# Attention and two expert layers on one core: first steps rearranged, and value products issued ahead of the next step's transposes

## The reference

```python
# q, k, v: (2, 8, 768, 64)   n_global = 8, n_local = 96
scores = (q @ k.T) / 8 - slope[h] * dist          # dist from position, n_local for global keys
scores = where(is_global | is_local, scores, -1e9)
a = softmax(scores);  x = (a @ v) -> (1536, 512)  # rows: batch and position, columns: heads
P = sinkhorn(exp(x @ w_gate))                     # 8 rounds over 1536 x 8
y = sum_e P[:, e] * (relu(x @ w1[e]) @ w2[e])     # 8 experts, 512 -> 1024 -> 512
out = one expert per row of y, 192 rows each, chosen in order of the logits
```

## Time and profile before

| what | value |
|---|---|
| median of 3 runs | 1588.49 us (1587.71 to 1588.54) |
| profiled execution | 1589.48 us, its span 1587.7 us |
| granted TensorE clock, mean over the span | 0.926 |
| busy share: TensorE, its weight loads, VectorE, ScalarE, GpSimd | 91%, 75%, 41%, 22%, 12% |
| chain that ended last, by engine | TensorE 87%, VectorE 7%, issue 3%, ScalarE 2% |
| share of that chain in L1232 to L1234 (expert layers) | 26%, 25%, 26% |
| L572, exponentials | 41.8 us in 96 |
| L829, bias | 34.5 us in 96 |

### The profile page before, as it was taken

How to read it: one execution, slowest core, us unless ns; L and a number is a source line. 1 busy time by engine, 2 the same in 40 slices (tenths; PEclk the granted TensorE clock), 3 DMA queues, 4 the chain that set the end, 5 groups by cost and what they waited for, 6 DMA issues and landing times.

```text
span 1587.7 us, 19242 instructions
## 1 busy us (share of the span) xinstructions
PE 1437.2 (91%) x7340; PEld 1187.6 (75%) x7340; DVE 655.0 (41%) x1572; ACT 343.6 (22%) x522; POOL 187.6 (12%) x176
## 2 busy tenths in 40 slices
PE   7997999999999999999999999999999233389997
PEld 4876788888888888888888888888886222278886
DVE  4365543232332332323323233232333888746663
ACT  2475212011021121211112202112112000034442
POOL 2242211011010110101101011010010200021210
PEclk7599999999999999999999999999999555589999
DMA  5552111010110101101011010010110300036660
GB/s 122 146 139 75 54 53 53 0 53 0 53 53 0 53 0 53 53 0 53 1 52 53 0 53 26 27 53 0 53 53 0 132 0 0 0 130 219 211 215 20
DMA packets 80021, 91.74 MB, mean 58 GB/s; under 512 B 36976, under 2 KB 43120, under 8 KB 79984
## 3 DMA queue, kind: packets, MB, share of 16 engines
q1 hardware_dynamic: 75024, 84.26, 16.7%
q0 software_dynamic: 2048, 6.29, 1.3%
q10 hardware_dynamic: 2912, 0.72, 0.3%
HBM read 84.97 MB, written 6.29 MB: 57 GB/s over the span
## 4 chain that ended last, share of the span: by engine, by line
PE 87%; DVE 7%; issue 3%; ACT 2%; POOL 0%; ACTq 0%; DMA 0%; DVEq 0%; POOLq 0%
PE PS L1232 26%; PE PS L1234 26%; PE PS L1233 25%; PE PS L1198 3%; PE PS L1324 2%; DVE G L989 1%; PE PS L1169 1%; PE PS L1179 1%; ACT sc L572 1%; PE PS L1246 0%; DVE xlo L849 0%; DVE thr L987 0%; PE PS L1347 0%; DVE lo L1000 0%; PE PS L1112 0%
## 5 line engine op out<-in xcount | busy, mean ns | idle before, releaser
L1232 PE MATMUL PS<-xhi,w1hi 128*128 128x512 f32 (+1 forms) x1024 | 372.0, 363 | 4.6 <-DVE hlo L855 3.2
L1233 PE MATMUL PS<-xlo,w1hi 128*128 128x512 f32 (+1 forms) x1024 | 370.8, 362 | 0.0
L1234 PE MATMUL PS<-xhi,w1lo 128*128 128x512 f32 (+1 forms) x1024 | 370.7, 362 | 0.0
L1232 PE MATMUL PS<-w2hi,hhi 128*128 128x512 f32 (+1 forms) x896 | 349.5, 390 | 0.0
L1234 PE MATMUL PS<-w2hi,hlo 128*128 128x512 f32 (+1 forms) x896 | 349.3, 390 | 0.0
L1233 PE MATMUL PS<-w2lo,hhi 128*128 128x512 f32 (+1 forms) x896 | 349.0, 390 | 0.0
L611 ACT ACTIVATE hhi<-PS 128x512 fp32r<-128x512 f32 (+1 forms) x256 | 135.6, 531 | 903.3 <-PE PS L1234 903.3
L855 DVE SCALAR_TENSOR_TENSOR hlo<-PS,hhi 128x512 fp32r<-128x512 f32 (+1 forms) x256 | 155.3, 607 | 409.3 <-ACT hhi L611 409.0
L868 DVE SCALAR_TENSOR_TENSOR acc<-PS,prob_e,acc 128x512 f32<-128x512 f32 x192 | 144.1, 750 | 352.2 <-PE PS L1234 352.0
L1232 PEld LDWEIGHTS PS<-xhi,w1hi 128*128 128x128 f32 x1024 | 194.8, 190 | 38.2 <-DVE hlo L855 4.0
L1233 PEld LDWEIGHTS PS<-xlo,w1hi 128*128 128x128 f32 x1024 | 194.8, 190 | 30.7
(11 more groups left out here) (193 smaller groups left out, 901.8 us busy)
## 6 DMA issues: line engine op xcount, KB each, us to landing
raw<-in_w SPq DMA_DIRECT2D x64, 1024.0 KB, 5.4
x_rows<-acc SPq DMA_DIRECT2D x3, 1024.0 KB, 10.6
vs<-in_v SPq DMA_DIRECT2D x14, 192.0 KB, 3.0
vw<-in_v SPq DMA_DIRECT2D x14, 120.0 KB, 2.9
qs<-in_qT SPq DMA_DIRECT2D x4, 384.0 KB, 4.0
kp<-in_kT SPq DMA_DIRECT2D x4, 384.0 KB, 4.9
raw<-in_qT SPq DMA_DIRECT2D x4, 384.0 KB, 4.2
raw<-in_kT SPq DMA_DIRECT2D x4, 384.0 KB, 5.0
```

The source lines that it names most:

```text
L1232: T.matmul(o, whi, xh, start=first, stop=False)
L1233: T.matmul(o, whi, xl, start=False, stop=False)
L1234: return T.matmul(o, wlo, xh, start=False, stop=last)
```

## The change

Three things. In the start: v of head 0 is loaded by SP, behind q and k of head 0 and ahead of q and k of head 1, instead of by ScalarE; ScalarE casts q and k of head 0 into qhi and khi, as soon as they have landed and ahead of the branch; VectorE subtracts both klo and qlo of head 0 behind its tables, and waits for ScalarE's table load only after that; GpSimd starts with head 1. The warming products are 50 instead of 46. In the loop: in every iteration the value products of step s-3 are issued ahead of the transposes of step s-2 instead of behind them. Waits and buffers of the loop are as they were.

```diff
@@ SP @@
-        def load_v(eng, h, par):
+            def load_v(h, par):
...
             load_qk(0)
+            sp.wait_ge(s_const, ONES_SET)
+            load_v(0, 0)
             load_qk(1)
-            sp.wait_ge(s_const, ONES_SET)
-            load_v(sp, 1, 1)
+            load_v(1, 1)
...
@@ GpSimd @@
-            for h in range(H):
+            for h in range(1, H):
                 pool.wait_ge(s_qh, 2 * h + 1)
                 pool.tensor_tensor(qlo[:, h % 2], q_raw[h % 2], qhi[:, h % 2].bitcast(F32), ALU.subtract).then_inc(s_ql, 1)
-                if h:
-                    pool.wait_ge(s_qh, 2 * h + 2)
-                    pool.tensor_tensor(own_pages(klo, h % 2), kp_flat[h % 2][:, P:], own_pages(khi, h % 2).bitcast(F32),
-                                       ALU.subtract).then_inc(s_ql, 1)
+                pool.wait_ge(s_qh, 2 * h + 2)
+                pool.tensor_tensor(own_pages(klo, h % 2), kp_flat[h % 2][:, P:], own_pages(khi, h % 2).bitcast(F32),
+                                   ALU.subtract).then_inc(s_ql, 1)
@@ ScalarE @@
-            act.wait_ge(s_const, ONES_SET)
-            load_v(act, 0, 0)
             act.wait_ge(s_const, H + 14)
 
             act.activation(negmax[:, 0:1], ident[:, 0:1], ACT.Exp).then_inc(s_tab, 1)
...
+            act.wait_ge(s_qk[0], 16 * QK_LOADS)
+            act.copy(qhi[:, 0], q_raw[0]).then_inc(s_qh, 1)
+            act.copy(own_pages(khi, 0), kp_flat[0][:, P:]).then_inc(s_qh, 1)
             path(act, lambda is_narrow: attend_window() if is_narrow else attend_full())
@@ VectorE @@
-            dve.wait_ge(s_tab, 1)
             m = [0]
...
-                if h == 0:
-                    dve.wait_ge(s_qh, 2)
-                    V.tensor_tensor(own_pages(klo, 0), kp_flat[0][:, P:], own_pages(khi, 0).bitcast(F32), ALU.subtract
-                                    ).then_inc(s_ql, 1)
+
+            def qk_lo_first():
+
+                dve.wait_ge(s_qh, 2)
+                V.tensor_tensor(own_pages(klo, 0), kp_flat[0][:, P:], own_pages(khi, 0).bitcast(F32), ALU.subtract
+                                ).then_inc(s_ql, 1)
+                V.tensor_tensor(qlo[:, 0], q_raw[0], qhi[:, 0].bitcast(F32), ALU.subtract).then_inc(s_ql, 1)
+                dve.wait_ge(s_tab, 1)
...
             def attend_window():
                 window_tables()
-                qk_hi(0)
+                qk_lo_first()
@@ TensorE @@
                 for s in range(STEPS + 7):
                     if s < STEPS:
                         scores(s)
+                    if 0 <= s - 3 < STEPS:
+                        products(s - 3)
                     if 0 <= s - 2 < STEPS:
                         transposes(s - 2)
-                    if 0 <= s - 3 < STEPS:
-                        products(s - 3)
...
-            spin(46)
+            spin(50)
```

More of the change, by code:

```diff
@@ L341, in load_qk @@
                              ).then_inc(s_qk[h % 2], 16)
+            def load_v(h, par):
+                vb = v[h].rearrange("(t p) (b d) -> p t b d", p=P, b=B)
+                for b in range(B):
+                    sp.dma_start(vs[:, par, :, b, 0:D], vb[:, :, b]).then_inc(s_vl[par], 16)
+                    sp.dma_start(vw[GK:P, par, :, b, 0:D], vb[GK:P, 0:QT - 1, b]).then_inc(s_vl[par], 16)
+                    sp.dma_start(vw[0:GK, par, :, b, 0:D], vb[0:GK, 0:1, b].to_broadcast([GK, QT - 1, D])
+                                  ).then_inc(s_vl[par], 16)
             def load_w1(e, half, par, u):
@@ L370, in _ @@
                 sp.wait_ge(s_ev, 2 * h - 1)
-                load_v(sp, h, h % 2)
+                load_v(h, h % 2)
             sp.wait_ge(s_ql, 2 * H)
```

## The result

The changed kernel took 1604.01 us, the median of 4 executions from 1599.97 to 1608.61; the kernel before took 1588.1 beside it. The ratio is 1.0107, interval 1.0071 to 1.0144: slower by 1.1% against these four executions of before. They were narrow by luck: 73 further executions of before, beside the experiments, have a median of 1589.4 us, and 15 of them took as long as the fastest of after; against that median the changed kernel is 0.9% slower. The forecast was 1573.8 with a range up to 1584, and 0.83 for faster. Ratios here leave out executions over 1.5% above the fastest of the same kernel, while medians are of all of them; the quotients of the medians differ from the ratios by 0.2% at most.

The account below looks back on a forecast made before the run. Attention's first 150 us set the gain: a chain at the start, then TensorE at half, later full clock. Start -5.0, clock -20.0 and order +10.3 sum to -14.7, giving 1573.8 us against the median; likely range 1560 to 1584.

Parts of the forecast that it names:

- What bounds the kernel: Attention, first 150 us: start a chain; heads 0 to 2 TensorE-bound at half clock, 3 to 7 at full clock.
- the forecast's two heads: Attention part: a head takes 20.44 us at half clock and 12.99 at full clock, 7.45 less.
- Part A: Start: shorter chain brings the first scores at 17.5 instead of 22.53 us, -5.0 us, bounds -4.0 to -5.4.
- the low value: Start: klo and qlo of head 0 together take 2.4 us on VectorE with GpSimd idle; upper bound 4.8.
- Part B: Heads 0 to 2: shorter TensorE gap keeps the clock at 2.4 GHz from the warming products; -20 us, bounds -17 and -21.
- rival (2): First steps: clock falls anyway, returns at the first x transposes; 1590.3 us, chance 0.12 shared with a late-start rival.
- -20.0 and +3.5: Heads 0 to 2: held clock saves 20 us; new order costs +2.7 in heads 1 and 2, +0.8 in head 0.
- rival (1): Attention loop: the new order costs nothing; -25 us, 1563.5, down to 1561; chance 0.21.
- Part C: Attention loop and drain: new order makes TensorE wait for ScalarE's copy, 2.23 us a step; +10.3 us, bounds -2 and +14.
- 3.8+0.8+2.7+0.8: New order's cost: heads 3 to 6, head 7 up to its last scores, heads 1 and 2, head 0.
- (3): Attention: as rival (2), but waits also keep the clock low past head 2; two heads make about 1603; chance 0.05.
- What would show it: Attention: right if clock stays 1.00 and steps near 2.23 us; wrong if clock 0.50 before the first x transposes.

Follow-up runs that it names:

- e15: Changed kernel with the old loop order and next head's q and k loaded ahead of v, no filler products; median 1573.1 us, 0.9906 of the kernel before.
- e14: e13 with the new loop order and 32 instead of 24 fillers in the first pause; median 1585.9 us, 0.9986 of the kernel before.
- e13: Changed kernel with old loop order, keys loaded ahead of v, first-expert weights late, fillers only in first steps and drain; 1564.30 us, 0.9843 of before.
- e7: Changed kernel with the old loop order, 24 filler products before the first value products and 4 in other steps; 1568.97 us, 0.9836 of before.
- e6: Changed kernel, new order kept, with 32 filler products before the first value products and 4 in other steps; 1573.85 us, 0.9874 of before.
- e2: Kernel before with only the loop order changed, old start kept; 1607.56 us, 1.0122 of the kernel before.
- e11: Changed kernel with the old loop order and a needless ScalarE copy ahead of each copy of the transposes; 1603.30 us, 1.0078 of before.
- e3: Changed kernel with eight filler products in every step, ahead of the wait for the copy; 1582.17 us, 0.9969 of the kernel before.
- e8: e7 with the first expert's weight loads behind the attention's loads and fillers in the drain and ahead of the gate; 1568.65 us, 0.9844 of before.
- e1: Changed kernel with the old loop order, so the new start alone; 1581.48 us, 0.9946 of the kernel before.

## Why the prediction was wrong

**What bounds the kernel** was read rightly, but from one execution. The kernel before is not a kernel of 1588 us. Beside these experiments it ran between 1572.34 (clock 0.938) and 1633.15 (0.890), with medians from 1589.21 to 1595.43 in five groups of 7 to 25. The three runs shown ahead of the prediction lay within 1 us of each other, and that was luck. The clock explains the spread: a span of 1570 us at a mean of 0.938 has 2 x 0.062 x 1570 = 195 us at half clock, one of 1631 at 0.890 has 359. That is 164 us more, and 61 us of time, 0.37 each; the forecast's two heads give (20.44-12.99)/20.44 = 0.36. And all of it lies in the attention part: over the 17 profiled executions the spans run from 1560.5 to 1618.4 us, and the part behind the gate only from 1430.4 to 1434.0.

**Part A** held: -4.3 against -5.0. klo took 1.63 us with GpSimd idle, 3.10 beside GpSimd's qlo; the low value was right, in agreement with the Trainium skill (GPSIMD Engine Reference, section 8, Key points). The first scores came 0.7 us later than forecast, behind the warming products, which ended at 18.26 and not at 17.1. The term that was mis-sized is theirs: "The granted clock was 1.00 while the warming products ran" is what the column says, but the first of them came every 0.43 us and only the later ones every 0.21, and how long the slow pace lasts differs from one execution to the next (to 7.72 in before, 10.28 in after, 8.13 in e15). The mean of 0.26 us of one execution could not price 50 in another. No load of head 1 was late.

**Part B failed**, and with it the forecast. The step is "So a pause of a microsecond between pieces of work is harmless here ... I expect the clock to stay at 2.4 GHz from the warming products on." It rested on the earlier trace rows, one stretch of one execution, and it passed over its own finding, that 2.5 us without work stand ahead of P(0); that was put into rival (2) and priced as if the load of head 1 had to be late for it. Measured, the pause was 2.06 us in after and 1.48 in the start alone, and the clock fell behind either. In other stretches 1.15 us (copies delayed) and 0.92 us (after, 88.5) were the last pause before a fall. No length of pause tells them apart: 1.48 us left the clock at 1.00 in e15, 0.92 us left it there twice more in after and four times in e14, and in before the pauses of the drain, 1.00, 1.07 and 1.25 us (up to 143.53, 147.91 and 150.24), left it at 1.00 as the forecast read it; it fell only near 154.5, late in a pause of 4.42. So "harmless here" was true of that stretch and did not carry over to others. Of the 27.7 us between the forecast and the profiled span, 17.1 arose up to S18, where the table has +0.6 and the forecast -20.0 and +3.5; 6.9 arose in head 4, and 3.5 in the drain. What is shown is the direction: fewer and shorter pauses hold the clock more often (e13, e7, e6), more and longer ones lose it more often (after, e2, e11), and work that computes nothing does as well as work that does. The -20 us was sized well: the held executions of the start alone (1566.27) and of e15 (1562.23) lie at rival (1)'s 1563.5, which is the sum of A and B (e15 has the keys first besides). It was the chance of it that was wrong.

**Part C** was right in mechanism and size, clock held: +8.1 up to the last scores, 2.23 a loop and +2.2 for the drain in e14, where the sum has 3.8+0.8+2.7+0.8 = 8.1, 2.23 and 2.2. That the sum meets so exactly is luck: by heads, e14 less e13, it is 4.5 for heads 3 to 6, 1.1 for head 7, 2.1 for heads 1 and 2 and 0.4 for head 0, so single terms are off by up to 0.7 either way. In after a pair of heads at full clock took 28.15, forecast 27.9. The drain came to 4.0 in after (9.73 less 5.70), as it ran in part at half clock. What it left out: the same 0.24 to 1 us waits that it added up are pauses of TensorE, and so they can cost a second time, through the clock. Of head 4's +7.9 the 6.9 beyond the forecast, and 3.5 of the +5.7 between S47 and the gate, are that second payment.

**The rivals.** What happened is (2) together with (3): the clock falls in the first steps, comes back at the first X, and one head beyond head 2 runs at half clock. (3) had 0.05. That 1604 is (3)'s "about 1603" is partly luck: (3) has the clock stay low for two heads more, while here it came back, was lost again for one head, and the drain gave the rest. (3) was argued away by "at half clock TensorE has no room for waits", which was true and beside the point: the loss comes at full clock. The rule of the Trainium skill (TensorE: Matmul & The Clock Gate, section A second HAM failure mode) said just this, brief idles between groups of matmuls swinging the clock, and the runs agree with it: e11 makes it happen in the old order, e3 and e6 stop it in the new one. One stretch of one trace was set against it, and that was too little.

**What would show it** did: a clock of 0.50 before the first X. A range to 1584 was too narrow even for an unchanged kernel.

**Open.** What exactly makes the clock fall or return; where the two longer executions of e14 and of e15 lose it; why the tail fillers of e8 gain nothing in the median.

## What to carry to other kernels

An edit that puts TensorE's next product behind a copy of its last one pays the wait once in time and often again in the clock. Price both, and give the second the larger chance. Where a kernel's mean granted clock is under 1, take several executions with their clocks before believing a median: three that agree say little. And the cheap remedy was not an order but steadiness: useless products in the first steps and the drain, and loads queued so that the keys do not wait behind another load's semaphore (1564.3 us, 1.6% faster than before, within 1 us).

## What the runs showed of the hardware

- The same program at the same point kept half clock for 54 us in one execution and 94 in another, with TensorE busy for over 99% of either. A dense stretch doesn't bring the clock back reliably.
- The same pause of 1.48 us in the same place was followed by a fall of the clock in one execution (e1) and not in another (e15); one of 0.92 us was followed by a fall once in after and not twice.
- The first warming products came every 0.43 us up to 7.7 us in one execution and up to 10.3 in another, then every 0.21, while the column of the granted clock read 1.00 throughout.
- 384 added products that compute nothing made the changed kernel 22 us faster (1604.0 to 1582.2).
- A VectorE subtraction of 1408 columns took 1.63 us alone and 3.10 beside one on GpSimd.
- In SyncE's queue a transfer that has its buffer waits for one ahead that has not: 2.64 us of VectorE and 2.18 of TensorE, once the attention part ran fast enough to meet it.
